# A fused attention, MoE and gated MoE kernel: the second MoE's x2 loaded and split one batch earlier, its first batch reordered, its last output by channel tiles

## What is computed

```python
def _moe2_ref(x, w_in, g_ln, w_sg, b_sg, w_out):
    h = gelu_tanh(x @ w_in)                       # 512 -> 1024
    u, v = h[..., :512], h[..., 512:]
    v_n = layer_norm(v) * g_ln                    # over channels
    v_s = einsum('ts,bsd->btd', w_sg, v_n) + b_sg[None, :, None]
    return x + (u * v_s) @ w_out                  # 512 -> 512
```

## Time and profile before

| | |
|---|---|
| median of 3 runs | 1297.19 us (1297.12 to 1297.50) |
| the profiled execution | 1298.31 us, span 1296.5 us |
| PE busy | 1263.0 us, 97% of the span |
| DVE, ACT, POOL busy | 849.5, 544.3, 101.4 us |
| second MoE, PE's part | 866 us to 1292 us of the span |

### The profile page before, as it was taken

One profiled execution on the slowest core, in us unless ns is written; L12 is line 12 of the kernel. 1 busy time (PEld: TensorE's weight loads), 2 busy tenths in 40 slices (PEclk: granted clock), 3 DMA queues, 4 the chain that ended last, 5 costly groups with the idle time before them and its releaser, 6 DMA issues.

```text
span 1296.5 us, 21575 instructions
## 1 busy us (share of the span) xinstructions
PE 1263.0 (97%) x8311; PEld 1221.2 (94%) x8311; DVE 849.5 (66%) x1196; ACT 544.3 (42%) x866; POOL 101.4 (8%) x107
## 2 busy tenths in 40 slices
PE   5699999999999999999999999999999999999998
PEld 5699999999999999999999999999899998998997
DVE  4886465645556558998888988976654655546443
ACT  4665454445455446544545444543222222222220
POOL 6210000000000000000000000002020211211100
PEclk9899999999999999999999999999999999999999
DMA  9555665555655466682735547272233141350421
GB/s 232 132 153 156 175 165 157 155 151 152 178 162 155 129 200 233 211 263 76 246 121 170 180 144 252 71 198 63 57 79 104 24 112 52 65 121 25 93 57 41
DMA packets 285365, 178.61 MB, mean 138 GB/s; under 512 B 197456, under 2 KB 255840, under 8 KB 285296
## 3 DMA queue, kind: packets, MB, share of 16 engines
q1 hardware_dynamic: 282336, 172.82, 46.3%
q0 software_dynamic: 1600, 4.56, 1.3%
q10 hardware_dynamic: 1360, 0.30, 0.1%
HBM read 109.47 MB, written 66.06 MB: 135 GB/s over the span
## 4 chain that ended last, share of the span: by engine, by line
PE 92%; DVE 3%; issue 2%; DMA 1%; SPq 1%; ACT 1%; POOL 0%; DVEq 0%; ACTq 0%; POOLq 0%
PE ps L1411 27%; PE ps L1413 27%; PE ps L1412 27%; PE ps L1432 3%; PE ps L1443 2%; PE ps L1416 2%; PE ps L1451 1%; PE ps L1462 1%; PE ps L1661 1%; PE ps L1660 1%; DMA wc_raw<-in_moe_w_out 1%; PE ps L1445 1%; DVE w_lo L1174 0%; SPq L375 0%; DVE vs L1349 0%
## 5 line engine op out<-in xcount | busy, mean ns | idle before, releaser
L1411 PE MATMUL ps<-x_hi,w 128*128 128x288 f32 x896 | 268.2, 299 | 3.7 <-DVE x_lo L1067 3.0
L1412 PE MATMUL ps<-x_lo,w 128*128 128x288 f32 x896 | 264.9, 296 | 0.0
L1413 PE MATMUL ps<-x_hi,w 128*128 128x288 f32 x896 | 264.5, 295 | 0.0
L1411 PE MATMUL ps<-r_hi,w_hi 128*128 128x384 f32 x672 | 224.8, 334 | 0.1
L1413 PE MATMUL ps<-r_hi,w_lo 128*128 128x384 f32 x672 | 224.7, 334 | 0.0
L1412 PE MATMUL ps<-r_lo,w_hi 128*128 128x384 f32 x672 | 224.6, 334 | 0.0
L877 ACT ACTIVATE r_hi<-hb 128x768 fp32r<-128x768 f32 x168 | 142.4, 848 | 168.6 <-PE ps L1413 164.8
L1411 PEld LDWEIGHTS ps<-x_hi,w 128*128 128x128 f32 x896 | 168.6, 188 | 5.9 <-issue 4.5
L1413 PEld LDWEIGHTS ps<-x_hi,w 128*128 128x128 f32 x896 | 169.0, 189 | 0.0
L1412 PEld LDWEIGHTS ps<-x_lo,w 128*128 128x128 f32 x896 | 168.7, 188 | 0.0
L1202 DVE TENSOR_TENSOR r_lo<-hb,r_hi 128x768 fp32r<-128x768 f32 x120 | 114.6, 956 | 29.7 <-ACT r_hi L877 29.7
(11 more groups left out here) (155 smaller groups left out, 2431.0 us busy)
## 6 DMA issues: line engine op xcount, KB each, us to landing
hT_scratch<-h_st SPq DMA_DIRECT2D x64, 576.0 KB, 4.6
hb<-hT_scratch SPq DMA_DIRECT2D x24, 1536.0 KB, 7.7
uT_scratch<-x_raw SPq DMA_DIRECT2D x32, 288.0 KB, 2.3
x_st<-uT_scratch SPq DMA_DIRECT2D x24, 384.0 KB, 3.7
x2T_scratch<-x_st SPq DMA_DIRECT2D x24, 384.0 KB, 7.0
x_raw<-x2T_scratch SPq DMA_DIRECT2D x8, 1152.0 KB, 5.8
xt_in<-x2T_scratch SPq DMA_DIRECT2D x144, 64.0 KB, 2.6
k_raw<-in_k SPq DMA_DIRECT2D x64, 128.0 KB, 4.0
```

The source lines that it names most:

```text
L1411: mm(dst, ws[0], xs[0], start=first, stop=False, skip_group_check=chained)
L1412: mm(dst, ws[0], xs[1], start=False, stop=False, skip_group_check=chained)
L1413: return mm(dst, ws[1], xs[0], start=False, stop=last, skip_group_check=chained)
```

## The change

The load of the next batch's x2 moves into `next_batch`, behind the first three blocks, so it is issued one batch sooner; ACT splits it at the start of an iteration in place of after the u tiles (batch 0 keeps its order). A one-element Gelu (`spare`) stands behind the last down product of the first MoE, where the w_out pieces were split; those now follow one each behind v tiles 1 to 4 of batch 0, on ACT and DVE. PE's wait for them moves to the first `spatial`. The w_sg pieces are transposed 2, 2, 2 in place of 1, 2, 3. PE's wait for the stacked tail moves to the matmul that reads it. The last batch's output goes through a new function, channel tile outermost, with its five position tiles in banks 0 to 4.

```diff
-        WS_AFTER = ((0,), (1, 2), (3, 4, 5), ())
+        WS_AFTER = ((0, 1), (2, 3), (4, 5), ())
...
-            def next_batch(p, par, q_, qpar):
+            def next_batch(p, par, q_, qpar, last=False):
 
                 load_first_blocks(p, par)
+                if not last:
+                    load_x2(*after(p, par))
                 store_out(q_, qpar)
                 stack_tail(p, par)
                 load_other_blocks(p, par)
 
             next_batch(0, 1, 0, 0)
-            with sp.Fori(0, B // 2 - 1) as i:
-
-                load_x2(i + 1, 0)
+            with sp.Fori(0, B // 2 - 2) as i:
+
                 next_batch(i + 1, 0, i, 1)
-                load_x2(i + 1, 1)
                 next_batch(i + 1, 1, i + 1, 0)
+            next_batch(B // 2 - 1, 0, B // 2 - 2, 1)
+            next_batch(B // 2 - 1, 1, B // 2 - 1, 0, last=True)
             store_out(B // 2 - 1, 1)
...
             down_tile(NTILE - 1, last=True)
-            for n in range(2 * DC, 3 * DC):
-                wc_high(n)
+            nc.scalar.activation(spare[:], eps_col[:], ACT.Gelu_apprx_tanh).then_inc(s_pass, 1)
...
             def iteration(p, par, first=False, last=False):
                 b = 2 * p + par
+                if not first and not last:
+                    x2_high(*after(p, par))
                 for c in range(DC):
...
-                if not last:
-                    x2_high(*after(p, par), first=first)
+                if first:
+                    x2_high(*after(p, par), first=True)
...
                     if j > VB[par]:
                         vn_high(p, par, j - 1, first)
+                    if first and j:
+                        wc_high(2 * DC + j - 1)
...
             x2_added(NTILE - 1, NI - 1)
-            for n in range(2 * DC, 3 * DC):
-                wc_low(n)
...
                     if j > VB[par] + 1:
                         low(j - 2)
+                    if first and j:
+                        wc_low(2 * DC + j - 1)
...
-            evacuate_others(B // 2 - 1, 1, start=0)
+            for i in range(batch_tiles(1)):
+                evacuate(B // 2 - 1, 1, i, bank=i)
...
+            def last_out_product(p, par):
+                tiles = batch_tiles(par)
+                for c in range(DC):
+                    pe.wait_ge(s_galo, DC * (2 * p + par) + c + 1)
+                    for i in range(tiles):
+                        if c == 0 and i == 2:
+                            pe.wait_ge(s_oev, NCP * p + OB[par])
+                        if c == 0 and i == JM:
+                            pe.wait_ge(s_vs, DC * (2 * p + par) + 3)
+                        js = slice(i * P, (i + 1) * P)
+                        ins = product(ps[:, i], [ga_hi[:, c, js], ga_lo[:, c, js]], [wo_hi[:, c, :], wo_lo[:, c, :]],
+                                      c == 0, c == DC - 1)
+                        if c == DC - 1:
+                            ins.then_inc(s_omm, 1)
...
                 pe.wait_ge(s_vnlo, NCP * p + VB[par + 1])
-                pe.wait_ge(s_vt, 32 * (b + 1))
...
                         mm(dst, vn_hi[:, JM, cs], ws_lo[:, JM + par, hs], start=False, stop=False)
+                        if c == 0 and h == 0:
+                            pe.wait_ge(s_vt, 32 * (b + 1))
                         ins = mm(dst, vt[:, cs], ws_hi[:, JM, hs], start=False, stop=True)
...
-            pe.wait_ge(s_wclo, 3 * DC)
+            pe.wait_ge(s_wclo, 2 * DC)
             pe.wait_ge(s_x2, NA2 * NTILE)
             u_product(0, 0, first=True)
             pe.wait_ge(s_wsb, 1)
+            pe.wait_ge(s_wclo, 3 * DC)
             spatial(0, 0)
...
-            out_product(B // 2 - 1, 1)
+            last_out_product(B // 2 - 1, 1)
```

More of the change, by code:

```diff
@@ L110, in build @@
     half_neg = at("half_neg", [P, 1], F32)
+    spare = at("spare", [P, 1], F32)
     low = cursor[0]
@@ L1363, in x2_transposed, with evacuate @@
                     nc.vector.transpose(o_st[i][:], xt_in[i % NXT][:]).then_inc(s_xtt, 1)
-            def evacuate(p, par, i):
+            def evacuate(p, par, i, bank=None):
                 j = OB[par] + i
@@ L1368, in evacuate @@
                 dve.wait_ge(s_xtt, NCP * p + j + 1)
-                nc.vector.tensor_tensor(o_st[i][:], ps[:, 2 + j % 2], o_st[i][:], ALU.add).then_inc(s_oev, 1)
+                nc.vector.tensor_tensor(o_st[i][:], ps[:, 2 + j % 2 if bank is None else bank], o_st[i][:], ALU.add).then_inc(s_oev, 1)
             def evacuate_others(p, par, start=1):
```

## The result

| | before | after |
|---|---|---|
| median | 1298.48 us (12 runs) | 1294.65 us (12 runs) |
| lowest to highest | 1296.44 to 1299.07 | 1293.79 to 1296.10 |
| the profiled execution | 1298.31, span 1296.5 | 1293.79, span 1292.0 |

The ratio is 0.9977, with a 95% interval of 0.9969 to 0.9985: 3.0 us faster, between 1.9 and 4.0. The two medians lie 3.8 us apart, which that interval holds too. The forecast was 3.45 us. The median of before is 1.3 us above that of the three runs that the prediction had, so it is the gain that is to be compared.

A forecast was written before the change was run, and what follows sets the result against it. PE, busy 97% of the span, was taken as the bound, so only its idle time and the work behind its last matmul could be won. 1.7 + 0.3 + 1.45 = 3.45 us, giving 1293.7 (own range 1293.0 to 1294.5; 8-in-10 1291.8 to 1295.6).

The forecast's parts named there:

- Part 1: Gate of batches 1, 3 and 5: x2 a stage sooner ends POOL's collision with DVE; 1.7 us gained, range 0 to 1.9.
- Rival A: Batches 2, 4 and 6: POOL's low part blocks output evacuations, PE stands 2.2 us three times, 6.6 us slower; chance 0.05.
- the one row at 903.13: Batch 0: a DVE operation reading PSUM and SBUF inside POOL's piece takes its normal 0.78 us, so evacuations should too.
- Part 2: Batch 0: moved table load and w_out pieces turn old waits into one of about 2.5 us; 0.3 us gained.
- the 1.49 and 0.98 us: Batch 0: PE's old waits for ACT's Gelu of a v tile and DVE's low part of a w_sg tile.
- the wait of 0.3 for Gelu 4: Batch 0: after channel tile 0 of u, w_sg tiles 0 and 1 wait 0.3 us for Gelu 4.
- Part 3: Last output product: channel tile outermost removes 1.6 us of gate waits; 1.45 us gained after queueing, bounds 0 to 1.6.
- The 0.15 for queueing: End of the kernel: 0.15 us taken off the last product's gain because all stores fall into 4 us.
- Rival B: End of the kernel: the burst of stores takes back the 1.45 us, giving 1295.2 us; chance 0.13.
- C: Batch 0 opens fully, pieces slip in beside the chain: 2.7 us more gained, 1291.0 us; chance 0.09.
- D: x2's split stays late and the gate keeps its collision: 1.7 us less gained, 1295.4 us; chance 0.06.
- E: Batch 0 loses 1.0 us in place of gaining 0.3, giving 1295.0 us; chance 0.07.

The follow-up runs named there:

- p1_load: The kernel before with only the early load of x2, ACT's split staying behind the u tiles; median 1296.56 us, ratio 0.9987.
- p1: The kernel before with only the early load and the early split of x2; median 1296.83 us, ratio 0.9988.
- after_c: The changed kernel, same source, executed once more; 1296.18 us (one execution), 33.66 us in batch 0.
- best: The changed kernel with the w_out pieces split two by two behind the first and second pair of w_sg pieces; median 1292.06 us, ratio 0.9953.
- after_b: The changed kernel, same source, executed once more; 1294.23 us (one execution), 32.12 us in batch 0.
- a_ws123: The changed kernel with the w_sg pieces in the old order 1, 2, 3; median 1296.40 us, ratio 0.9986.
- p2: The kernel before with only the batch 0 changes (Gelu table, w_out pieces, w_sg pieces 2, 2, 2) and the moved wait; median 1297.12 us, ratio 0.9994.
- p3: The kernel before with only the last output product by channel tiles, evacuated from banks 0 to 4; median 1296.30 us, ratio 0.9986.

## Why the prediction was right, and where it was thin

**Part 1, 1.7 us: measured 1.74, for a partly wrong reason.** The number was read from one execution, and there it is exact. The stated chain (POOL blocks a DVE operation with two SBUF inputs, the next vs is late, PE waits) holds. What the prediction did not see is that the price depends on the few tenths of a us between the starts of POOL and DVE: over the five profiled executions with the late load it was 1.7 twice, 1.5, 0.7 and 0 (what the stretch has above the 376.63 to 376.66 of those without a wait). The bounds said 0 to 1.9, for another reason. That the full 1.7 came out of this pair of traces is partly luck: the mean of the five is 1.1, which with 0.53 and 1.6 makes 3.3 us (an estimate from these profiles), nearer to the 3.0 timed than the 3.9 of the two traces. And the early load does the work alone (p1_load); that the split's move would do it without the early load was not run.

**Rival A, blocked evacuations: did not happen,** as the one row at 903.13 had said; p1 and after show 0.69 us for each evacuation beside POOL's piece.

**Part 2, 0.3 us: measured 0.53.** The step that mattered, the 1.49 and 0.98 us turned into a new wait at w_sg piece 2, came out as 2.14 for 2.5. The terms that were off: the chain took 3.48 us per tile (877.89 to the next Gelu at 881.37), not 3.6, since a piece adds 0.51; the last vn_high came at 886.17, not 887.1 (0.6 of that is the earlier start of the stage); and the wait of 0.3 for Gelu 4 did not appear. What was missing is the half clock behind the new wait, 1.5 us in after_c: the sum priced a wait by its length only. The traces differ by more than the timing says: 4.5 us of span, of which 3.9 in the changed stretches and 0.6 ahead of them, against 3.0 timed. The half clock can be a part of that, the phase of the gate another; besides, the profiled execution of after is the fastest of its twelve.

**Part 3, 1.45 us: measured 1.6.** The PE side was right to 0.01 us. The 0.15 for queueing was not needed: from the last evacuation to the end it is 4.1 us in both. Rival B found no support: six stores issued within 3.9 us ended as soon as the last tile's alone, though for two of these us the DMA engines were busy all the time (the first of the two in after, DMA share and GB/s last):

```profile
1287.00:1288.00 1.00, 0.86 (x4) 0.38 (x2) 1.00 (x3) 0.00 (x0) 0.00 (x0) 1.00 1.01 379
```

The Trainium skill gives 2 us for an HBM access at high load ("DMA: Bandwidth & Descriptors", Latency and other measured facts); nothing of that size is seen here at 379 GB/s.

**The others.** C, batch 0 opens fully, was the right size for another kernel: best shows 3.0 us (32.64 - 29.64), once the pieces leave the chain. D fell with the stage column. E's lost us exists (after_c's 33.66 is 1.0 above before's 32.64), as the half clock, but not by the mechanism named.

The measured median, 1294.65, lies in the 8-in-10 range, 0.15 us above the forecast's own range and above the 1294.6 that was to count as faster by over 0.2%. That line was drawn from a median of 1297.19; by the ratio the gain is 0.23%, and its interval reaches both sides of 0.2%. With before at 1298.48 the forecast gain of 3.45 us would have meant 1295.0.

## What to carry to other kernels

When an edit removes a wait, follow the chain of the other engines to the next semaphore that the bottleneck asks for: here small work pushed between the links of an ACT and DVE chain (0.5 us each, four times) turned two waits of 1.5 and 1.0 into one of 2.1, and placing the same work behind the chain was worth more than the rest of the change's part in that batch. A stall that one trace shows may be a matter of phase; look for how close the two starts lie before its price is put into a sum. And a wait of the bottleneck can cost more than its length, by the clock that follows it: here in two profiles of six.

## What the runs showed of the hardware that I had not expected

- Behind one and the same PE wait of 2.16 us the granted clock of TensorE stayed at 1.00 in after_b and fell to 0.50 for 3.4 us in after_c, 1.4 us behind the wait's end; in a_ws123 it fell 0.8 us behind it and cost 1.6 us. Over 2.14 to 2.16 us of wait in six profiles it fell in these two.
- POOL's subtraction with two SBUF inputs holds up DVE's operation with two SBUF inputs to its own end (0.76 becomes 3.0 to 6.3 us); which operation is hit is a matter of phase, since a start of POOL 1.4 us later let the first multiplication pass and caught the second (p2). Where DVE was first by 0.05 and 0.3 us, POOL's piece was the longer one, 6.29 and 6.04 us in place of 5.7 (p2 batch 3, p3 batch 1). Operations that read one input from PSUM kept their time (evacuations 0.69, vs from PSUM 0.78 to 0.82). The Trainium skill ("SBUF — State Buffer", Who interferes with whom) says that a DVE instruction with two SBUF inputs contends with a GpSimd instruction that reads SBUF, and one with at most one SBUF input does not. The traces agree.
- Six stores of 1.31 MB in all, issued within 3.9 us, took no longer to the end of the span than one tile's two (4.1 us behind the start of the last evacuation in both).
